# Attention scores written in one burst over four PSUM banks, the upper and lower halves of pairs formed from SBUF, and a new order of a step's work on TensorE and ScalarE

## The chip, the cores and the metric

The kernel runs on one core of a Trainium2 chip. The metric is the device time of one execution in microseconds (us); less is better. The engines are called as the profile calls them: PE (TensorE; PEld is its weight load), DVE (VectorE), ACT (ScalarE), POOL (GpSimd) and SP (the engine that only issues DMAs here).

## What is computed

Three stages, all in fp32:

```
scores = scale * q @ k^T                     # 4 batches x 8 heads, 576 x 576, head size 64
kth    = 32nd largest score of each row      # scores below it are masked out
attn   = softmax(masked scores);  a = attn @ v
x      = a as (2304 tokens, 512)
y      = relu(x @ w_in)**2 @ w_out           # 512 -> 2048 -> 512
out    = y + gate * (relu(y_e @ w1[e]) @ w2[e])   # for tokens with y @ w_skip > 0,
                                             # e = expert (of 8) with the largest logit y @ w_gate
```

## The kernel before

**Tiling.** The attention is 72 steps. A step takes 128 query rows against all 576 keys, for two heads at once (`n` = 0, 1 in the code): 64 steps of kind "pair" and 8 of kind "mixed", which gather the last 64 rows of each head. Eight steps make a group of 256 tokens, so there are 9 groups. The MLP (x to y) runs on a group in 16 units `u` of 128 hidden columns; each unit is `up(u)` (12 matmuls of 256 columns) and, two units later, `down(u)` (6 matmuls of 512 columns). The high and low part of each operand are separate fp32r tiles, which is why there are three products for one. When all y are there, tokens are routed and the experts run tile by tile; the change does not touch that stage.

**One step on the engines.** PE multiplies q and k (`scores_half`, two halves of 288 key columns for both heads). ACT copies each half, scaled, from PSUM to the tile `s_sb` (a ring of 4). DVE finds the 32nd largest value of each row. To halve its work it first forms, from the two halves of a row, the elementwise larger (`upper`) and smaller (`lower`) values, 576 elements each for the two heads (`find_upper`, `find_lower`; one operand is the second half still in PSUM, the other the first half in `s_sb`), and then runs rounds of MAX8 and MATCH_REPLACE8 on them. `mins` and `kth` close a step's search. POOL turns kth into a bias (`set_bounds`), ACT computes from it what lies below (`find_below`), POOL subtracts that (`mask`), ACT exponentiates, DVE inverts the sums (`invert_sums`), POOL multiplies by them (`normalise`), PE transposes the probabilities (`transpose_probs`), ACT copies them back (`copy_transposed`, 1152 columns), PE multiplies by v (`values_product`), and ACT and POOL split the result into x_high and x_low (`copy_values`, `split_x`). For a unit of the MLP, ACT takes relu and g_high, POOL the square and g_low (`square_low`: L644 and L649).

**What sets the order.** No scheduler does: each engine has its own program, written out by hand as a loop over t = 0 to 86, and runs it strictly in that order; semaphores join the engines. In iteration t an engine works on different steps at once. POOL, for instance, does bounds of step t-1, normalise of t-2, split_x of t-3, mask of t-1, then, for t = 1 to 13, its share of splitting the MLP's weights into high and low (`split_out_low` L657, `split_in_low` L664: four pieces at t = 1, three each at t = 2 to 9, one each at t = 10 to 13), then the squares of the two MLP units of t. The MLP runs from t = 10, two units an iteration. In iteration t DVE finishes the search of step t, and forms upper and lower of step t+1 between its third and its fourth round.

PE's iteration before is: first half of the scores of t+1, values of t-3, second half of the scores of t+1, transposes of t-2, both MLP units, and, three times for each group, a share of the routing (`transpose_y`, `route_parts`, `route`). Both halves of the scores use banks 0 and 1 of PSUM in turn, so the second half waits for ACT's copy of the first, and the next step's first half waits until DVE has formed `lower` from the second (the wait on `lower_set`). Transposes use banks 2 to 4, the values part of bank 4, MLP units banks 5 to 7.

## Time and profile before

| | us |
|---|---|
| median of 3 runs | 922.72 |
| lowest and highest of them | 922.64, 923.32 |
| span of the profiled execution | 920.5 |
| of it: attention alone, t = 0 to 9 | about the first 105 |
| of it: attention and MLP together | about 105 to 697 |
| of it: rest of the MLP, routing | about 697 to 790 |
| of it: experts | about 790 to 920 |

A row in order of time gives the start and length in us, the engine, the line, the operation, the tiles it writes and reads with their shapes, and how many equal instructions were merged into it. A row of a group by line gives the count, the busy time, the mean length in ns, then the time for which the engine stood idle before such an instruction and what released it. Matmul lengths overlap, so the distance between starts tells more than their length.

### The profile page before, as it was taken

What the parts mean: (1) busy time and instruction counts of PE and PEld (TensorE: products, weight loads), DVE (VectorE), ACT (ScalarE), POOL (GpSimd) and SP (SyncE); (2) the same over time, 40 slices, a digit from 0 to 9 for tenths busy, and PEclk for the clock granted to TensorE, in tenths of its full rate; (3) what the DMA queues carried; (4) which work ended last, traced back from release to release, by engine and by line L of the source; (5) the groups of instructions that cost most, each with busy time, mean ns of one, the idle gap of its engine ahead of it and who ended that gap; (6) DMA issues with size and microseconds to landing.
All of it is one profiled execution on the core that took longest, in us unless ns stands there. A gap on an engine that the chain in (4) does not pass through costs nothing.

```text
span 920.5 us, 21085 instructions
## 1 busy us (share of the span) xinstructions
PE 885.1 (96%) x6684; PEld 719.2 (78%) x6684; DVE 819.2 (89%) x2584; ACT 658.5 (72%) x1297; POOL 656.6 (71%) x884
## 2 busy tenths in 40 slices
PE   4799899999999999999999999999999999999997
PEld 2677687888888788888788887888878886788886
DVE  6999999999999999999999999999991064888887
ACT  3777787777777778777777777877775322788886
POOL 2999998878887787787888778778787452444432
PEclk7799999999999999999999999999999999999999
DMA  9962533566344658866535455433533675764990
GB/s 332 364 242 95 173 125 124 166 203 193 120 166 142 212 181 280 239 188 229 170 130 169 138 186 171 169 125 125 189 125 114 242 243 208 273 226 154 335 334 23
DMA packets 69750, 175.40 MB, mean 191 GB/s; under 512 B 21298, under 2 KB 26418, under 8 KB 65280
## 3 DMA queue, kind: packets, MB, share of 16 engines
q1 hardware_dynamic: 67568, 168.77, 54.2%
q0 software_dynamic: 1840, 5.06, 1.7%
q8 instruction: 56, 0.92, 0.4%
q14 instruction: 62, 0.51, 0.2%
q10 hardware_dynamic: 224, 0.15, 0.1%
HBM read 154.19 MB, written 21.27 MB: 191 GB/s over the span
## 4 chain that ended last, share of the span: by engine, by line
PE 84%; DVE 11%; POOL 2%; issue 1%; ACT 1%; DMA 0%; DVEq 0%; SPq 0%; POOLq 0%
PE psum L1352 8%; PE psum L1417 7%; PE psum L1418 7%; PE psum L1419 7%; PE psum L1377 7%; PE psum L1434 7%; PE psum L1435 7%; PE psum L1396 7%; PE psum L1436 7%; DVE top L1052 3%; DVE upper L1057 3%; PE psum L1650 2%; PE psum L1619 2%; PE psum L1624 2%; PE psum L1655 2%; PE psum L1658 2%
## 5 line engine op out<-in xcount | busy, mean ns | idle before, releaser
L1052 DVE MAX8 top<-upper 128x8 f32<-128x288 f32 x576 | 238.8, 446 | 0.0
L629 POOL TENSOR_TENSOR s_sb<-s_sb,below 128x576 f32<-128x576 f32 x144 | 203.3, 1434 | 1.5 <-ACT below L801 1.5
L1057 DVE MATCH_REPLACE8 upper<-top,upper 128x288 f32<-128x288 f32 x432 | 187.6, 441 | 0.0
L1417 PE MATMUL psum<-x_high,w_in_high 128*128 128x256 f32 x576 | 168.3, 292 | 1.6 <-POOL x_low L635 1.1
L1418 PE MATMUL psum<-x_low,w_in_high 128*128 128x256 f32 x576 | 161.8, 281 | 0.0
L1419 PE MATMUL psum<-x_high,w_in_low 128*128 128x256 f32 x576 | 161.2, 280 | 0.0
L792 ACT ACTIVATE s_sb<-psum 128x576 f32<-128x576 f32 x144 | 93.8, 651 | 93.7 <-PE psum L1352 84.2
L644 POOL TENSOR_TENSOR square<-relu 128x256 f32<-128x256 f32 x144 | 89.7, 623 | 81.7 <-ACT relu L834 80.9
L649 POOL TENSOR_TENSOR g_low<-square,g_high 128x256 fp32r<-128x256 f32 x144 | 108.4, 753 | 30.3 <-POOL square L644 23.2
L1352 PE MATMUL psum<-k_sb,q_sb 64*128 64x288 f32 x512 | 100.1, 469 | 21.7 <-DVE lower L1043 19.1
L801 ACT ACTIVATE below<-s_sb,steep_kth 128x576 f32<-128x576 f32 x144 | 110.8, 770 | 9.2 <-POOL neg_max L617 8.4
L1067 DVE MAX8 top<-lower 128x8 f32<-128x288 f32 x288 | 115.3, 441 | 0.0
L1434 PE MATMUL psum<-w_ring,g_high 128*128 128x512 f32 x288 | 114.5, 398 | 0.0
L1435 PE MATMUL psum<-w_ring,g_high 128*128 128x512 f32 x288 | 113.5, 394 | 0.0
L1436 PE MATMUL psum<-w_ring,g_low 128*128 128x512 f32 x288 | 113.2, 393 | 0.0
L1417 PEld LDWEIGHTS psum<-x_high,w_in_high 128*128 128x128 f32 x576 | 108.5, 188 | 6.0 <-POOL x_low L635 1.3
L1418 PEld LDWEIGHTS psum<-x_low,w_in_high 128*128 128x128 f32 x576 | 108.7, 189 | 3.2
L809 ACT ACTIVATE s_sb<-s_sb,neg_max 128x576 f32<-128x576 f32 x144 | 110.9, 770 | 0.0
L834 ACT ACTIVATE relu<-psum 128x256 f32<-128x256 f32 x144 | 55.5, 385 | 76.1 <-PE psum L1419 75.0
L1419 PEld LDWEIGHTS psum<-x_high,w_in_low 128*128 128x128 f32 x576 | 108.6, 189 | 0.0
L623 POOL TENSOR_SCALAR s_sb<-s_sb,sums 128x576 f32<-128x576 f32 x144 | 106.3, 749 | 0.0
L1377 PEld LDWEIGHTS psum<-ident,s_sb 128*128 128x128 f32 x576 | 62.1, 142 | 34.0 <-issue 30.2
(213 smaller groups left out, 1848.0 us busy)
## 6 DMA issues: line engine op xcount, KB each, us to landing
w_ring<-w_split SPq DMA_DIRECT2D x144, 512.0 KB, 4.5
weights<-w SPq DMA_DIRECT2D x32, 1024.0 KB, 7.1
v_sb<-v_main SPq DMA_DIRECT2D x48, 256.0 KB, 2.5
w_split<-w_ring SPq DMA_DIRECT2D x16, 512.0 KB, 4.3
k_sb<-kT SPq DMA_DIRECT2D x32, 144.0 KB, 4.5
k_sb<-kT SPq DMA_DIRECT2D x32, 128.0 KB, 4.3
weights<-w_out SPq DMA_DIRECT2D x1, 4096.0 KB, 13.5
weights<-w_in SPq DMA_DIRECT2D x1, 4096.0 KB, 21.1
```

Source lines behind the costliest of these rows:

```text
L629: nc.gpsimd.tensor_tensor(s_sb[:, s % SBUFS, n, 0:S], s_sb[:, s % SBUFS, n, 0:S], below[:, n, :], ALU.subtract).then_inc(masked, 1)
L1052: v.max(top[:, s % 2, n, 8 * r:8 * r + 8], upper[:, s % 2, n, :]).then_inc(upper_step, 1)
L1057: v.match_replace(upper[:, s % 2, n, :], top[:, s % 2, n, 8 * r:8 * r + 8], upper[:, s % 2, n, :], LOWEST).then_inc(upper_step, 1)
L1067: v.max(top[:, s % 2, n, at:at + 8], lower[:, s % 2, n, :]).then_inc(lower_step, 1)
L1352: last = t_.matmul(banks[:, n, :], q_sb[own, a % RING_A, r * P:(r + 1) * P], k_sb[own, a % RING_A, cols], start=True, stop=True)
L1377: t_.transpose(psum[:, 2 + n, k * P:(k + 1) * P], tiles[:, at:at + P], ident[:, :])
L1417: t_.matmul(dst, wh, x_high[:, j % 2, k, :], start=k == 0, stop=False)
L1418: t_.matmul(dst, wh, x_low[:, j % 2, k, :], start=False, stop=False)
L1419: last = t_.matmul(dst, wl, x_high[:, j % 2, k, :], start=False, stop=k == KC - 1)
L1434: t_.matmul(psum[:, 6 + c, :], gh, wh, start=f == 0, stop=False)
L1435: t_.matmul(psum[:, 6 + c, :], gh, wl, start=False, stop=False)
L1436: last = t_.matmul(psum[:, 6 + c, :], gl, wh, start=False, stop=f == FT - 1)
```

## The change

The scores of a step are now written in one burst, half 0 to banks 0 and 1, half 1 to banks 2 and 3, with one semaphore count for the step. ACT copies them in one instruction of 1152 columns (only step 0 is copied by halves). `find_upper` and `find_lower` take both operands from `s_sb` and are plain tensor_tensor max and min. PE no longer waits for `lower_set`; in turn the transposes, which use banks 2 and 3 too, wait until ACT has copied the scores of the step three further on (`scores_copied`), and the burst waits for the copy of the previous transposes. PE's iteration is now: scores of t+1, first MLP unit, routing share, transposes of t-2, second MLP unit, values of t-2. ACT's order follows. The first `up` of a group waits for its last x_low only at its last slice of k. The routing's tiles move from banks 2 and 3 to 0 and 1.

```diff
-        def score_banks(s, half):
-            at = 2 if s == 0 and half == 1 else 0
-            return psum[:, at:at + 2, 0:HALF]
+        def score_banks(half):
+            return psum[:, 2 * half:2 * half + 2, 0:HALF]
...
+            def copy_scores(s):
+                act.wait_ge(scores_done, s + 2)
                 if s >= SBUFS:
                     act.wait_ge(transposed, s - SBUFS + 1)
+                nc.scalar.activation(s_sb[:, s % SBUFS, :, :].rearrange("p n (h c) -> p n h c", h=2),
+                                     psum[:, 0:4, 0:HALF].rearrange("p (h n) c -> p n h c", h=2), ACT.Copy,
+                                     scale=SCALE).then_inc(scores_copied, 1)
...
-                if t + 1 < NS:
-                    copy_scores(t + 1, 0)
+                if 0 <= t - 3 < NS:
+                    copy_values(t - 3)
                 if 0 <= t - 1 < NS:
                     find_below(t - 1, 0)
-                if 0 <= t - 3 < NS:
-                    copy_values(t - 3)
+                    find_below(t - 1, 1)
                 if t + 1 < NS:
-                    copy_scores(t + 1, 1)
...
+                    copy_scores(t + 1)
...
-                v.scalar_tensor_tensor(out=upper[:, s % 2, :, :], in0=score_banks(s, 1), scalar=SCALE,
-                                       in1=s_sb[:, s % SBUFS, :, 0:HALF], op0=ALU.mult, op1=ALU.max).then_inc(upper_set, 1)
+                v.tensor_tensor(upper[:, s % 2, :, :], s_sb[:, s % SBUFS, :, HALF:S], s_sb[:, s % SBUFS, :, 0:HALF], ALU.max
+                                ).then_inc(upper_set, 1)
...
-                v.scalar_tensor_tensor(out=lower[:, s % 2, :, :], in0=score_banks(s, 1), scalar=SCALE,
-                                       in1=s_sb[:, s % SBUFS, :, 0:HALF], op0=ALU.mult, op1=ALU.min).then_inc(lower_set, 1)
+                v.tensor_tensor(lower[:, s % 2, :, :], s_sb[:, s % SBUFS, :, HALF:S], s_sb[:, s % SBUFS, :, 0:HALF], ALU.min
+                                ).then_inc(lower_set, 1)
...
             def transpose_probs(s):
+                pe.wait_ge(scores_copied, min(s + 3, NS - 1) + 2)
                 wait(pe, transposed_copied, s)
+                wait(pe, values_copied, s)
...
+                whole = KC - 1 if ORDER[j] else KC - 2
                 if f == 0:
-                    pe.wait_ge(x_low_done, PER_GROUP * (j + 1))
+                    pe.wait_ge(x_low_done, PER_GROUP * (j + 1) - (2 if ORDER[j] else 1))
...
                 for k in range(KC):
+                    if f == 0 and k == whole:
+                        pe.wait_ge(x_low_done, PER_GROUP * (j + 1))
```

The change's instructions on PE, for a step in which the MLP runs, in the order of its program. Before, L1352 is a score matmul, L1396 the values, L1377 and L1380 the transposes, L1417 the first matmul of an MLP unit, L1434 the first of its second half:

```order
L1352 MATMUL psum<-k_sb,q_sb 128x288 [waits lower_set,scores_copied,kq_loaded0]
L1352 MATMUL psum<-k_sb,q_sb 128x288
L1396 MATMUL psum<-pT_sb,v_sb 64x128 [waits v_loaded2,values_copied,transposed_copied]
L1396 MATMUL psum<-pT_sb,v_sb 64x128 x7
L1396 MATMUL psum<-pT_sb,v_last 64x128 x2
L1352 MATMUL psum<-k_sb,q_sb 128x288 [waits scores_copied]
L1352 MATMUL psum<-k_sb,q_sb 128x288
L1377 MATMUL psum<-ident,s_sb 128x128 [waits probs_done,transposed_copied]
```

After (the same operations are L1353, L1412, L1395, L1438 and L1455; the second piece follows the first MLP unit, the third the second one):

```order
L1353 MATMUL psum<-k_sb,q_sb 128x288 [waits transposed_copied,scores_copied,kq_loaded0]
L1353 MATMUL psum<-k_sb,q_sb 128x288 x3
L1438 MATMUL psum<-x_high,w_in_high 128x256 [waits relu_done]
...
L1395 MATMUL psum<-ident,s_sb 128x128 [waits values_copied,probs_done,transposed_copied,scores_copied]
L1395 MATMUL psum<-ident,s_sb 128x128 x3
L1395 MATMUL psum<-ident,s_sb 128x128 [waits probs_done]
...
L1412 MATMUL psum<-pT_sb,v_sb 64x128 [waits v_loaded2,values_copied,transposed_copied]
```

The two bursts of scores have become one, the transposes stand in the middle of the MLP's work, and they carry a new wait, on `scores_copied`.

On DVE the place of `upper` and `lower` in the program is the same, with other operands. Before:

```order
L1036 SCALAR_TENSOR_TENSOR upper<-psum,s_sb 128x576 [waits upper_step,scores_copied]
L1043 SCALAR_TENSOR_TENSOR lower<-psum,s_sb 128x576 [waits lower_step]
L1052 MAX top<-upper 128x8 [waits upper_step] x2
L1095 RECIPROCAL sums<-sums 128x2 [waits exp_done]
L1052 MAX top<-upper 128x8 [waits upper_set,bias_set]
```

After:

```order
L1046 TENSOR_TENSOR upper<-s_sb 128x576 [waits upper_step,scores_copied]
L1053 TENSOR_TENSOR lower<-s_sb 128x576 [waits lower_step]
L1062 MAX top<-upper 128x8 [waits upper_step] x2
L1105 RECIPROCAL sums<-sums 128x2 [waits exp_done]
L1062 MAX top<-upper 128x8 [waits upper_set,bias_set]
```

Nothing moved here; both inputs are now in SBUF.

On ACT a plain iteration after the change reads as follows (L836 and L837 copy the values, L810 finds what lies below kth, L794 copies the scores, L845 is relu, L818 the exponential, L854 g_high, L827 copies the transposes):

```order
L836 ACTIVATE x_now<-psum 128x128 [waits x_low_done,values_done]
L837 ACTIVATE x_high<-psum 128x128
L810 ACTIVATE below<-s_sb,steep_kth 128x576 [waits masked,bias_set]
L810 ACTIVATE below<-s_sb,steep_kth 128x576 [waits masked]
L794 ACTIVATE s_sb<-psum 128x1152 [waits transposed,scores_done]
L845 ACTIVATE relu<-psum 128x256 [waits squared,unit_up]
L818 ACTIVATE s_sb,sums<-s_sb,neg_max 128x576 [waits probs_done,masked]
L854 ACTIVATE g_high<-relu 128x256 [waits g_low_done,unit_down,relu_done]
L827 ACTIVATE pT_sb<-psum 128x1152 [waits values_done,transposed]
L818 ACTIVATE s_sb,sums<-s_sb,neg_max 128x576 [waits probs_done,masked]
```

Before, the iteration began with the first half of the scores, and the copy of the transposes stood ahead of the first relu:

```order
L792 ACTIVATE s_sb<-psum 128x2x288 [waits transposed,scores_done]
L801 ACTIVATE below<-s_sb,steep_kth 128x576 [waits masked,bias_set]
L825 ACTIVATE x_now<-psum 128x128 [waits x_low_done,values_done]
...
L792 ACTIVATE s_sb<-psum 128x2x288 [waits transposed,scores_done]
L801 ACTIVATE below<-s_sb,steep_kth 128x576 [waits masked]
L816 ACTIVATE pT_sb<-psum 128x1152 [waits values_done,transposed]
L834 ACTIVATE relu<-psum 128x256 [waits squared,unit_up]
```

What moved is that the one copy of the scores now stands behind both `find_below`, so the transposes on PE that wait for it also wait for the kth of that iteration.

## Rows read from the trace of the kernel before

**Rows 1.** Groups by line, 200 to 600: busy us, mean ns; idle before, releaser.

```profile
L649 POOL TENSOR_TENSOR g_low<-square,g_high 128x256 fp32r<-128x256 f32 x83 | 61.1, 737 | 21.7 <-POOL square L644 18.5
...
L644 POOL TENSOR_TENSOR square<-relu 128x256 f32<-128x256 f32 x83 | 51.3, 618 | 39.7 <-ACT relu L834 39.7
...
L816 ACT ACTIVATE pT_sb<-psum 128x1152 f32<-128x1152 f32 x42 | 47.4, 1128 | 0.0
...
L1036 DVE SCALAR_TENSOR_TENSOR upper<-psum,s_sb 128x576 f32<-128x576 f32 x42 | 31.4, 749 | 0.0
...
L1095 DVE RECIPROCAL sums<-sums 128x2 f32<-128x2 f32 x42 | 6.8, 162 | 8.0 <-ACT s_sb L809 8.0
```

**Rows 2.** Stretch 200:300: length, then PE, PEld, DVE, ACT, POOL, clock, DMA.

```profile
200.00:300.00 100.00, 100.00 (x789) 81.91 (x787) 98.62 (x347) 76.41 (x164) 80.37 (x114) 1.00 0.50 163
```

**Rows 3.** In order of time, one step with an MLP: start, length (us), instruction.

```profile
407.12 0.17 DVE L1090 TENSOR_REDUCE kth<-mins 128x2 f32<-128x34 f32 x1
...
411.13 2.83 POOL L629 TENSOR_TENSOR s_sb<-s_sb,below 128x576 f32<-128x576 f32 x2
...
413.50 0.75 DVE L1036 SCALAR_TENSOR_TENSOR upper<-psum,s_sb 128x576 f32<-128x576 f32 x1
...
416.57 0.17 DVE L1090 TENSOR_REDUCE kth<-mins 128x2 f32<-128x34 f32 x1
```

**Rows 4.** In order of time, DVE, a step before the MLP starts.

```profile
65.95 0.16 DVE L1090 TENSOR_REDUCE kth<-mins 128x2 f32<-128x34 f32 x1
...
72.33 0.73 DVE L1036 SCALAR_TENSOR_TENSOR upper<-psum,s_sb 128x576 f32<-128x576 f32 x1
72.99 0.73 DVE L1043 SCALAR_TENSOR_TENSOR lower<-psum,s_sb 128x576 f32<-128x576 f32 x1
...
74.81 0.17 DVE L1083 TENSOR_TENSOR mins<-top 128x34 f32<-128x34 f32 x1
...
75.27 0.16 DVE L1090 TENSOR_REDUCE kth<-mins 128x2 f32<-128x34 f32 x1
```

**Rows 5.** In order of time, POOL, the same step.

```profile
66.20 0.19 POOL L615 TENSOR_SCALAR steep_kth<-kth 128x2 f32<-128x2 f32 x1 [0.65 <-DVE kth L1090]
...
68.37 2.80 POOL L629 TENSOR_TENSOR s_sb<-s_sb,below 128x576 f32<-128x576 f32 x2
71.12 3.75 POOL L664 TENSOR_TENSOR w_in_low<-weights,w_in_high 128x512 fp32r<-128x512 f32 x3
```

**Rows 6.** In order of time, DVE and POOL, second step.

```profile
23.23 4.96 POOL L657 TENSOR_TENSOR w_ring<-weights,w_ring 128x512 fp32r<-128x512 f32 x4
...
27.21 1.03 DVE L1083 TENSOR_TENSOR mins<-top 128x34 f32<-128x34 f32 x1
...
28.54 0.16 DVE L1090 TENSOR_REDUCE kth<-mins 128x2 f32<-128x34 f32 x1
```

**Rows 7.** In order of time, DVE and POOL, routing after the attention.

```profile
750.50 2.29 DVE L1206 TENSOR_TENSOR place_hit<-s_sb,row_iota 128x2048 f16<-128x2048 f32 x1
...
751.81 1.45 POOL L644 TENSOR_TENSOR square<-relu 128x256 f32<-128x256 f32 x1 [1.39 <-ACT relu L834]
...
752.82 0.47 DVE L1207 CAST ahead_values<-s_sb 128x16 f16<-128x16 f32 x1
```

**Rows 8.** By form, 800 to 920: subtraction with both operands in SBUF.

```profile
L1283 DVE TENSOR_TENSOR w_low<-weights,w_high 128x1024 fp32r<-128x1024 f32 x39 | 47.1, 1246 | 2.3 <-ACT w_high L982 2.3
```

**Rows 9.** In order of time, PE, the step at 407.

```profile
410.06 0.76 PE L1352 MATMUL psum<-k_sb,q_sb 64*128 64x288 f32 x4
410.75 1.09 PE L1377 MATMUL psum<-ident,s_sb 128*128 128x128 f32 x8
```

**Rows 10.** In order of time, PE, start of the kernel.

```profile
4.38 2.01 PE L1352 MATMUL psum<-k_sb,q_sb 64*128 64x288 f32 x8 [0.30 <-DMA k_sb<-kT]
...
10.19 1.33 PE L1352 MATMUL psum<-k_sb,q_sb 64*128 64x288 f32 x4 [0.74 <-ACT s_sb L792]
```

More of the change, by code:

```diff
@@ L508, in _ @@
                     if FREED[a - RING_A] == t:
-                        sp.wait_ge(scores_done, 2 * t + 2)
+                        sp.wait_ge(scores_done, t + 2)
                         load_kq(a)
@@ L937, in _ @@
                     square_high(u)
+                if 0 <= t - 2 < NS:
+                    copy_transposed(t - 2)
                 if 0 <= t - 1 < NS:
                     exponentiate(t - 1, 1)
+                for j in range(GROUPS - 1):
+                    if ENDS[j] == t:
+                        copy_yT(j)
+                    if ENDS[j] + 1 == t:
+                        copy_parts(j)
+                    if ENDS[j] + 2 == t:
+                        copy_logits(j)
                 for u in slots[1:2]:
@@ L943, in _ @@
                 for j in range(GROUPS):
[L944 to L949 removed]
+                    if ENDS[j] - 1 == t:
+                        copy_rows(j)
+                if t == ENDS[GROUPS - 1]:
+                    copy_yT(GROUPS - 1)
                 if t == ENDS[GROUPS - 2] + 3:
@@ L1338, in scores_half @@
                 kind, _, _, _, r, a = STEPS[s]
-                if half == 0:
-                    for x in range(a, a + (1 if kind == "pair" else 2)):
-                        pe.wait_ge(kq_loaded[x % RING_A], KQ_COUNT[x])
-                if s > 0:
-                    pe.wait_ge(scores_copied, 2 * s + half)
-                if half == 0:
-                    wait(pe, lower_set, s)
-                banks = score_banks(s, half)
                 cols = slice(half * HALF, (half + 1) * HALF)
@@ L1351, in scores_half @@
                         own = slice(n * HD, (n + 1) * HD)
-                        last = t_.matmul(banks[:, n, :], q_sb[own, a % RING_A, r * P:(r + 1) * P],
+                        last = t_.matmul(psum[:, 2 * half + n, 0:HALF], q_sb[own, a % RING_A, r * P:(r + 1) * P],
                                          k_sb[own, a % RING_A, cols], start=True, stop=True)
@@ L1448, in transpose_y @@
                     for k in range(KC):
-                        last = t_.transpose(psum[:, 2 + c, k * P:(k + 1) * P], rows[:, j % 2, c, k * P:(k + 1) * P], ident[:, :])
+                        last = t_.transpose(psum[:, bank + c, k * P:(k + 1) * P], rows[:, j % 2, c, k * P:(k + 1) * P], ident[:, :])
                     if j == GROUPS - 1 and c == 0:
@@ L1513, in _, with routing_share @@
             keep_clock(5)
-            scores_half(0, 0)
-            scores_half(0, 1)
+            def routing_share(t):
+                for j in range(GROUPS - 1):
+                    if ENDS[j] == t:
+                        transpose_y(j)
+                    if ENDS[j] + 1 == t:
+                        route_parts(j)
+                    if ENDS[j] + 2 == t:
+                        route(j)
+            scores(0)
             for t in range(TIMES):
@@ L1518, in _ @@
                 if t + 1 < NS:
-                    scores_half(t + 1, 0)
-                if 0 <= t - 3 < NS:
-                    values_product(t - 3)
-                if t + 1 < NS:
-                    scores_half(t + 1, 1)
-                if 0 <= t - 2 < NS:
-                    transpose_probs(t - 2)
+                    scores(t + 1)
                 if 2 <= t < FIRST:
                     keep_clock(20)
+                if not slots and 0 <= t - 2 < NS:
+                    transpose_probs(t - 2)
                 for u in slots:
@@ L1536, in _ @@
                         last.then_inc(ahead_transposed, 1)
+                    if u % 2 == 0:
+                        routing_share(t)
+                        if 0 <= t - 2 < NS:
+                            transpose_probs(t - 2)
+                if 0 <= t - 2 < NS:
+                    values_product(t - 2)
                 if t == ENDS[GROUPS - 1]:
@@ L1542, in _ @@
                     up_ahead(0, [0])
-                for j in range(GROUPS):
-                    if ENDS[j] == t:
-                        transpose_y(j)
-                    if ENDS[j] + 1 == t and j < GROUPS - 1:
-                        route_parts(j)
-                    if ENDS[j] + 2 == t and j < GROUPS - 1:
-                        route(j)
+                    transpose_y(GROUPS - 1)
                 if t == ENDS[GROUPS - 1] + 1:
```

81 lines of the change are left out of this document (41 added, 40 removed).

## The prediction

> **What bounds the kernel now.** I read first the stretches, then the groups by line, then one step in order of time. Between 200 and 600 us, where attention and MLP run together, three engines are close to full: PE 100 us of 100, DVE 98.6, POOL 80.4 [rows 2]. The count of `upper` gives the pace: 42 in 400 us, 9.52 us a step on average, plain steps and those with a routing share together [rows 1]. A plain step is 9.45 us, from 407.12 to 416.57 [rows 3]. DVE stands still for only 8.0 us of the 400, before the inversion of the sums [rows 1], 0.19 us a step. So DVE needs 9.52 - 0.19 = 9.33 us for its own work. The first ten steps, without MLP, confirm it: there kth follows kth after 75.27 - 65.95 = 9.32 us [rows 4] with no idle time on DVE. So DVE bounds the first 105 us, PE bounds the next 590 by a hair, and whatever lengthens DVE's step by more than 0.19 us becomes the bound everywhere. After 697 us PE's MLP and then the experts bound; the change leaves these stages alone, and I cost them at nothing.
>
> **The scores on PE.** A half of the scores takes from 410.06 to 410.75, 0.69 us, before the next operation may start [rows 9], two halves 1.38. A burst in one piece stands in the trace once, in step 0 at the lower clock: 2.01 us for eight against 1.33 for four [rows 10], which take 0.76 at the full one [rows 9]. The second four added 0.68 there, and at twice the clock I take 0.34. So the burst costs 0.69 + 0.34 = 1.03, a saving of 0.35 us a step; the ends are 0 (no saving) and 0.45 (the second half costs a third of the first). PE's own work falls from 9.52 to 9.17 on average. Against that stands one new stall. The first `up` of a group needs x_low of step t-3, which POOL now makes in the same iteration, behind bounds and normalise, about 2.3 us after kth. PE reaches that `up` about when kth ends, and its first three quarters last about 1.1 us, so it waits some 1.3 us once in 8 steps, 0.16 a step. PE: 9.33, as much as DVE.
>
> **Upper and lower on DVE.** Their length hardly changes. An operation with both operands in SBUF takes 0.17 us for 34 elements (`mins`, rows 4) and 2.29 for 2048 [rows 7]; on the line between them 1024 elements take 1.21 (measured: 1.246 on average, some of it waiting [rows 8]) and 576 take 0.74, against 0.749 before [rows 1]. The Trainium skill, page "VectorE: DVE Perf Modes", section on the TRN2 errata, gives 120 cycles ahead of the elements for a PSUM source and 58 for SBUF; by that each would be 0.06 us shorter, an estimate of 0.13 a step and 8 us in all if nothing but DVE counted. The row disagrees and decides.
>
> **What DVE and POOL do to each other.** In this trace a DVE operation with two SBUF inputs and a POOL operation do not run together. `mins` of the second step starts at 27.21, while POOL's four splits last from 23.23 to 28.19 [rows 6]; it takes 1.03 us instead of 0.17, and ends about when POOL's fourth ends. That step's kth starts 0.86 us late. It holds the other way too: POOL's square, 618 ns otherwise [rows 1], starts at 751.81 under a `place_hit` that ends at 752.79 and takes 1.45 [rows 7]; and the DVE operation behind, at 752.82, takes 0.47 for 16 elements, while that square runs. So the port changes hands between two DVE operations when POOL has waited. The lost time is the overlap less about 0.13 us. `upper` with one operand in PSUM pays nothing: at 413.50 it runs under `mask` (411.13 to 413.96) for 0.46 us and takes 0.75 as ever [rows 3]. The change gives it a second SBUF operand.
>
> The Trainium skill says the same in "SBUF — State Buffer", section "Who interferes with whom": a DVE instruction with two SBUF inputs contends with a GpSimd one that reads SBUF, and whichever starts first holds the port for its whole length. By this rule the trace agrees.
>
> **Steps without MLP (t = 1 to 9).** Times from the end of kth (66.11): POOL starts at +0.09, ends `mask` at +5.06, and then runs three splits 1.25 apart, to +8.76 [rows 5]; `upper` asks at +6.22, `lower` at +6.88, `mins` at +8.70 [rows 4]. The first split ends at +6.28, which costs `upper` nothing. The second asked at +6.26, after `upper`, and gets the port when `upper` lets it go, at +6.84; it ends at about +8.09, so `lower`, asked at +6.88, loses 8.09 - 6.88 - 0.13 = 1.08. `mins` then asks at +9.78, and the third split is over by then but for its tail. A step costs 9.32 + 1.08. Bounds: without any change of hands POOL still has to fit in 8.67 us of its own and 2 x 0.62 of DVE's, about 10.0, that is +0.67 less what slack absorbs, say +0.3; if the second split came just before `upper` (0.04 us apart), two splits are lost, +2.2. I take 1.08, the one that the order of requests gives: 8 steps of three splits 8.6 us, t = 1 with four another 1. At t = 10 to 13 one split and two MLP units: POOL's 5.0 + 1.3 + 2.7 and DVE's 1.2 give 10.2 against 9.4, 4 x 0.8 = 3. Sum 13 (4 to 22).
>
> **Steps with MLP (58 further ones).** DVE is the later engine, so the rest falls in place behind kth. POOL: `mask` ends at +5.09. ACT: both `find_below` end at +1.9, the scores' copy (1152 columns as pT's, 1128 ns, rows 1) at +3.0, relu at +3.3, the exponential waits for `mask` and ends at +4.5, g_high at +4.9. POOL squares from +5.05 to +5.66 and makes g_low from +5.74 to +6.47 (618 and 737 ns, rows 1). `upper` asks at +6.22 and loses 6.47 - 6.22 - 0.13 = 0.12. PE's transposes start at +3.0 behind the copy and end at +4.2; ACT copies them until +6.0, exponentiates until +6.8, and gives the second relu at +7.05. POOL asks for its square at +7.13, `lower` at +7.0: `lower` is first and loses nothing; the square waits until +7.6, g_low follows until +9.04, `mins` asks at +8.82 and loses 0.09. The step is 9.33 + 0.21 = 9.54. A routing share, three in eight steps, puts up to 1.0 us more on ACT between exponential and second relu, which moves the last g_low under `mins` and past the next kth; I add 0.08 on average. 9.62 against 9.52: 58 x 0.10 = 6 us.
>
> **Sum.** 922.7 + 13 + 6 = 941.7. The profiled execution has a span of 920.5, 2.2 under the median; what lies around the span is unchanged, so the sum goes on the median. Forecast 941 us, own range 928 to 953.
>
> **Rivals.** *Faster.* The requests fall into POOL's gaps (between +6.47 and +7.13 there is one of 0.66 us), or the port is held through both operations, so that what remains is PE's saving: a step then takes the larger of DVE's 9.33 and PE's 9.17 to 9.33. 62 x 0.17 = 10 us less, plus at most 4 early: 913 to 917. For it: the gap exists and ACT's order could place it well. Against it: PE's and ACT's work now hangs on kth through the scores' copy, so POOL's chain keeps its place, and the early steps have no gap at all. *Much slower.* In the MLP steps `lower` comes behind the second unit's square instead of ahead of it. They are 0.13 us apart, and the waits of `upper` push `lower` that way. Then each step loses 0.48 more: 58 x 0.48 = 28, so 969; half of the steps, 955. It decides where `lower` asks later than POOL's second square. The x_low stall and the routing shares, which make PE late, push the square the other way, but under `mins`. *No slowing at all by the port*, because these operations' forms differ from the ones seen: rows 6 and 7 show three forms and both directions, so I hold this for unlikely; it is the faster case. *The change doesn't do what it says* (DVE no longer holding PE): it can't move the steady state, since PE's wait for `lower` is already zero there.
>
> **How the numbers follow.** Forecast 0.52; much slower (953 and above) 0.20; faster 0.22; gains and port losses cancelling 0.06, split over the middle. A measurement of this kernel can tell about 0.2% (1.8 us) from no change. Faster 0.24, same 0.04, slower 0.72. The range goes from 915 to 965: it cuts the lower half of the faster case and the end of the much slower one.
>
> **What will show it.** Right: `upper`, `lower` and `mins` well above 0.75, 0.75 and 0.17 us on average, `lower` near 1.8 in the steps before 100 us; kth to kth about 10.4 us there and 9.6 later; POOL's operations of a step longer by 0.1 to 0.6; PE with idle time ahead of the transposes, released by ACT's copy of the scores; eight score matmuls in about 1.03. Wrong: upper and lower at 0.75 throughout, and a pace of 9.33. It would be wrong in size if the steps with the MLP lock in another order of square and `lower`, or if PE, late by its stall, sets the pace instead of DVE.

## The result, and the profile of the changed kernel

| us | before | changed |
|---|---|---|
| median (lowest, highest), 4 runs each | 923.02 (922.64, 923.47) | 933.89 (933.32, 934.18) |
| span of the profiled execution | 920.5 | 931.5 |
| start of kth, step 0 | 18.35 | 18.11 |
| start of kth, step 9 | 103.25 | 109.94 |
| start of kth, step 13 | 140.56 | 151.07 |
| start of kth, step 71 (the last) | 694.97 | 709.40 |

The changed kernel is slower: ratio 1.0117, 95% interval 1.0103 to 1.0131. The forecast was 941 with a range of 915 to 965.

The starts of kth split the 11.0 us between the two spans. Steps 1 to 9 cost 6.9 more, steps 10 to 13 cost 3.8 more, the 58 steps from 14 to 71 cost 3.9 more (9.626 against 9.559 us a step), the start is 0.2 shorter, and what follows the last kth is 3.4 shorter (222.1 against 225.5).

**The bound has moved to DVE.** First a stretch. The columns are the stretch and its length, the busy time of PE, PEld, DVE, ACT and POOL with their instructions, the granted clock of PE, the share of DMA and GB/s:

```profile
200.00:300.00 100.00, 98.99 (x785) 82.01 (x784) 100.00 (x344) 75.33 (x152) 81.83 (x115) 1.00 0.51 168
```

In [rows 2] PE was the engine without a gap and DVE had 98.6 of 100. Now DVE has no gap, here and in the three stretches up to 600 us, and PE has one of a per cent. The chain that ended last (the work followed back from the last instruction, as shares of the span), in the page of the kernel before and then of the changed one, says the same with other means:

```profile
PE 84%; DVE 11%; POOL 2%; issue 1%; ACT 1%; DMA 0%; DVEq 0%; SPq 0%; POOLq 0%
```

```profile
DVE 66%; PE 27%; issue 5%; DVEq 0%; ACT 0%; DMA 0%; POOL 0%; SPq 0%
```

**Which operations grew.** The groups by line from 200 to 600 us, to be laid beside [rows 1]; the last two numbers ahead of the second bar are busy us and mean ns, behind it stands idle time and its releaser:

```profile
L650 POOL TENSOR_TENSOR g_low<-square,g_high 128x256 fp32r<-128x256 f32 x82 | 62.5, 762 | 6.4
...
L645 POOL TENSOR_TENSOR square<-relu 128x256 f32<-128x256 f32 x82 | 57.8, 705 | 52.1 <-ACT relu L845 52.1
...
L1046 DVE TENSOR_TENSOR upper<-s_sb 128x576 f32<-128x576 f32 x41 | 37.3, 909 | 0.0
...
L1053 DVE TENSOR_TENSOR lower<-s_sb 128x576 f32<-128x576 f32 x41 | 33.3, 812 | 0.0
...
L1093 DVE TENSOR_TENSOR mins<-top 128x34 f32<-128x34 f32 x41 | 10.5, 256 | 0.0
```

`upper` went from 749 to 909 ns, its elements being the same, and `lower` has 812. On the other side of the port `square` went from 618 to 705 ns and `g_low` from 737 to 762. All these operations have the same sizes as before, so the excess is waiting that the profile counts as length.

**The early steps alternate.** From step 1 on, kth follows kth after 10.63, 11.15, 9.33, 10.92, 9.33, 10.91, 9.34, 10.89 and 9.33 us. Before, it followed after 10.19 and 9.42 in the first two of these steps, in which `mins` waited for POOL [rows 6], and after 9.32 or 9.33 from the third on [rows 4]. Two neighbouring steps of the changed kernel in order of time, DVE and POOL together. First the long one:

```profile
95.45 4.76 POOL L665 TENSOR_TENSOR w_in_low<-weights,w_in_high 128x512 fp32r<-128x512 f32 x3
...
96.10 1.23 DVE L1046 TENSOR_TENSOR upper<-s_sb 128x576 f32<-128x576 f32 x1
97.25 1.82 DVE L1053 TENSOR_TENSOR lower<-s_sb 128x576 f32<-128x576 f32 x1
...
100.61 0.17 DVE L1100 TENSOR_REDUCE kth<-mins 128x2 f32<-128x34 f32 x1
100.87 0.19 POOL L616 TENSOR_SCALAR steep_kth<-kth 128x2 f32<-128x2 f32 x1 [0.67 <-DVE kth L1100]
```

and then the short one:

```profile
105.79 5.00 POOL L665 TENSOR_TENSOR w_in_low<-weights,w_in_high 128x512 fp32r<-128x512 f32 x3
...
106.99 0.75 DVE L1046 TENSOR_TENSOR upper<-s_sb 128x576 f32<-128x576 f32 x1
107.66 0.75 DVE L1053 TENSOR_TENSOR lower<-s_sb 128x576 f32<-128x576 f32 x1
...
109.94 0.17 DVE L1100 TENSOR_REDUCE kth<-mins 128x2 f32<-128x34 f32 x1
```

Inside each merged row of three splits (the splitting of the MLP's weights, L665), the second one is what matters. A view of 97.3 to 98.6 shows the second and third of the long step, the second starting at 96.67; in a view of 108.3 to 109 the second of the short step stands alone:

```profile
96.67 3.53 POOL L665 TENSOR_TENSOR w_in_low<-weights,w_in_high 128x512 fp32r<-128x512 f32 x2
```

```profile
107.01 2.53 POOL L665 TENSOR_TENSOR w_in_low<-weights,w_in_high 128x512 fp32r<-128x512 f32 x1
```

In the long step `upper` asks at 96.10, while the first split runs (95.45 to 96.70), and loses 0.49 us. The second split is let in behind `upper`, and `lower` loses 1.07. In the short step the first split is over when `upper` starts (it ends about 107.06, 0.07 of overlap); `upper` and `lower` both run at 0.75, and it is the second split that waits through both: 2.53 us instead of 1.27. POOL is then late. Its three splits end at 110.79, 0.85 us behind the start of kth, where it otherwise begins its next chain 0.26 us behind kth (100.87 after 100.61). So its chain for the next step starts late, its first split falls under the next `upper`, and the next step is a long one. The control below (e2_after_struct) supports this: in its step 5 DVE waited 1.75 us for ACT, POOL caught up meanwhile, and there two short steps followed each other.

### The profile page after: what moved, and what is told of

The parts are those of the page before. It is cut to its first block, busy times and chain, and to the rows that moved or that the text cites. A ratio compares the mean times of both kernels' runs of the same rounds, so it can differ in the third digit from the quotient of the medians.

```text
span 931.5 us, 21036 instructions
## 1 busy us (share of the span) xinstructions
PE 879.7 (94%) x6684; PEld 726.0 (78%) x6684; DVE 844.6 (91%) x2584; ACT 648.2 (70%) x1226; POOL 681.3 (73%) x884
## 4 chain that ended last, share of the span: by engine, by line
DVE 66%; PE 27%; issue 5%; DVEq 0%; ACT 0%; DMA 0%; POOL 0%; SPq 0%
DVE top L1062 21%; DVE upper L1067 18%; DVE top L1077 9%; DVE upper L1046 6%; DVE lower L1082 6%; DVE lower L1053 3%; PE psum L1679 2%; PE psum L1648 2%; PE psum L1653 2%; PE psum L1684 2%; PE psum L1687 2%; PE psum L1657 2%; PE psum L1438 2%; PE psum L1455 2%; PE psum L1457 2%
## 5 line engine op out<-in xcount | busy, mean ns | idle before, releaser
L1438 PE MATMUL psum<-x_high,w_in_high 128*128 128x256 f32 x576 | 175.2, 304 | 8.3 <-POOL x_low L636 8.3
L645 POOL TENSOR_TENSOR square<-relu 128x256 f32<-128x256 f32 x144 | 102.5, 712 | 92.6 <-ACT relu L845 89.7
L810 ACT ACTIVATE below<-s_sb,steep_kth 128x576 f32<-128x576 f32 x144 | 103.9, 771 | 62.4 <-POOL neg_max L618 60.8
L1438 PEld LDWEIGHTS psum<-x_high,w_in_high 128*128 128x128 f32 x576 | 108.5, 188 | 35.9 <-issue 25.4
L818 ACT ACTIVATE s_sb<-s_sb,neg_max 128x576 f32<-128x576 f32 x144 | 110.9, 770 | 27.8 <-POOL s_sb L630 27.7
L650 POOL TENSOR_TENSOR g_low<-square,g_high 128x256 fp32r<-128x256 f32 x144 | 112.9, 784 | 11.3
L1455 PE MATMUL psum<-w_ring,g_high 128*128 128x512 f32 x288 | 113.8, 395 | 0.0
L827 ACT ACTIVATE pT_sb<-psum 128x1152 f32<-128x1152 f32 x72 | 81.2, 1128 | 29.3 <-PE psum L1396 28.5
L1353 PE MATMUL psum<-k_sb,q_sb 64*128 64x288 f32 x512 | 83.5, 446 | 13.1 <-ACT s_sb L794 11.9
L1412 PE MATMUL psum<-pT_sb,v_sb 128*64 128x128 f32 x1024 | 72.0, 284 | 13.4 <-ACT pT_sb L827 13.4
L1412 PEld LDWEIGHTS psum<-pT_sb,v_sb 128*64 128x64 f32 x1024 | 56.1, 139 | 36.0 <-issue 20.0
```

The source lines that it names most:

```text
L650: nc.gpsimd.tensor_tensor(g_low[:, u % RING_G, :], square[:, :], g_high[:, u % RING_G, :].bitcast(F32), ALU.subtract).then_inc(g_low_done, 1)
L1412: last = t_.matmul(values_psum[hd * HD:(hd + 1) * HD, :], v_part, pT_sb[:, at:at + P], start=k == 0, stop=k == KT - 1)
L1438: t_.matmul(dst, wh, x_high[:, j % 2, k, :], start=k == 0, stop=False)
L1455: t_.matmul(psum[:, 6 + c, :], gh, wh, start=f == 0, stop=False)
```

## The experiments

Each set of runs shared a chip and the runs of the kernel before, whose median was 922.82 us beside the first four and 922.65 beside the last two. "Kernel before" and "changed kernel" below are the two of this document. Where an edit only changes where a wait or an operation stands, its diff is cut to that.

**The operands alone (e1_before_sbuf).** The kernel before with the changed operands of `upper` and `lower`, and nothing else of the change:

```diff
-                v.scalar_tensor_tensor(out=upper[:, s % 2, :, :], in0=score_banks(s, 1), scalar=SCALE,
-                                       in1=s_sb[:, s % SBUFS, :, 0:HALF], op0=ALU.mult, op1=ALU.max).then_inc(upper_set, 1)
+                v.tensor_tensor(upper[:, s % 2, :, :], s_sb[:, s % SBUFS, :, HALF:S], s_sb[:, s % SBUFS, :, 0:HALF], ALU.max
+                                ).then_inc(upper_set, 1)
```

(and `lower` with min in the same way)

> The kernel before, with only upper and lower taken from SBUF (tensor_tensor max and min); order and banks as before. Theory A (two SBUF operands make DVE and POOL exclude each other, and that is the loss): slower than before, first ten steps as in the changed kernel (+7 us by t = 9), some 3 more to t = 13, then 0.1 to 0.3 us a step over 58 steps: 933 to 950 us, point 940; upper about 1.25 and lower 1.8 in every second early step. Theory B (the new order, with PE and ACT hanging on kth, is the loss, and SBUF operands cost nothing): 923 us as before, upper and lower 0.75.

Measured: 935.97 us, ratio 1.0142 (1.0125 to 1.0159). Span 935.1. With this edit alone the kernel loses at least as much as with the whole change: 13.2 us against 10.9, though the two intervals overlap. The alternation is there too, with the same lengths, in two neighbouring steps of this kernel (DVE in order of time):

```profile
97.30 1.24 DVE L1036 TENSOR_TENSOR upper<-s_sb 128x576 f32<-128x576 f32 x1
98.46 1.81 DVE L1043 TENSOR_TENSOR lower<-s_sb 128x576 f32<-128x576 f32 x1
...
108.20 0.74 DVE L1036 TENSOR_TENSOR upper<-s_sb 128x576 f32<-128x576 f32 x1
108.86 0.75 DVE L1043 TENSOR_TENSOR lower<-s_sb 128x576 f32<-128x576 f32 x1
```

So PE's new order and the burst are not what makes the kernel slow. After the last kth (709.00) this kernel takes 226.1 us, as the one before does (225.5); the 3.4 us that the changed kernel wins there don't come from its being bound by DVE, since this kernel is bound by DVE too.

**A control (e2_after_struct), and the one factor reversed (e3_after_psum).** `upper` and `lower` can't simply read PSUM in the changed kernel, since the routing and PE's next work would overwrite it. The control has the changed kernel's burst, order and SBUF operands, but PE's burst waits for `lower` again, the routing's tiles are back in banks 2 and 3 and its share, on PE and on ACT, stands behind the second MLP unit. Of this the diff shows PE's part:

```diff
                 if s > 0:
                     pe.wait_ge(scores_copied, s + 1)
+                    wait(pe, lower_set, s)
+                last = scores_half(s, 0)
+                if s > 0:
                     wait(pe, transposed_copied, s - 3)
...
-                last = scores_half(s, 0)
                 if s == 0:
                     last.then_inc(scores_done, 1)
...
                     if u % 2 == 0:
-                        routing_share(t)
                         if 0 <= t - 2 < NS:
                             transpose_probs(t - 2)
+                routing_share(t)
                 if 0 <= t - 2 < NS:
                     values_product(t - 2)
```

> The changed kernel with PSUM laid out so that half 0 of the scores could stay in banks 0 and 1 until DVE has read it: routing tiles back in banks 2 and 3, the routing share behind the second MLP unit, PE's burst waits for lower again. Operands of upper and lower still from SBUF. It is the control for the next kernel. Theory A and B both: as the changed kernel, 934 us, within 3.

Measured: 933.68, ratio 1.0111 (1.0094 to 1.0128), the same as the changed kernel within 0.3 us. In the two traces the stages differ more than the sum: steps 1 to 9 take 1.9 us longer in the control (one of them with that wait of DVE for ACT), steps 10 to 13 take 1.0 less and the 58 behind them 1.3 less. In sum, what PE was freed from, waiting for `lower`, is worth nothing measurable while DVE sets the pace.

The next kernel differs from the control in `upper` and `lower` only: one of their two operands is the first half of the scores, still in PSUM, and since it isn't scaled yet, the instruction is a scalar_tensor_tensor.

```diff
-                v.tensor_tensor(upper[:, s % 2, :, :], s_sb[:, s % SBUFS, :, HALF:S], s_sb[:, s % SBUFS, :, 0:HALF], ALU.max
-                                ).then_inc(upper_set, 1)
+                v.scalar_tensor_tensor(out=upper[:, s % 2, :, :], in0=score_banks(0), scalar=SCALE,
+                                       in1=s_sb[:, s % SBUFS, :, HALF:S], op0=ALU.mult, op1=ALU.max).then_inc(upper_set, 1)
```

> The same as the control, but upper and lower take half 0 from PSUM and half 1 from SBUF (scalar_tensor_tensor), so one operand in SBUF; all results as in the reference. Theory A: the waits at the port go, kth to kth falls to 9.33 us in every stretch, upper and lower 0.75 us; what is left is PE's saving: 912 to 917 us, faster than before and than the control by some 20. Theory B: no change against the control, 931 to 937 us, although upper and lower have 0.75.

Measured: 915.61, ratio 0.992 (0.9903 to 0.9937). This is 18.1 us less than the control, and it beats both kernels. (As in the first run, `lower` is changed with `upper`, with min.) The groups by line from 200 to 600 us show where they went:

```profile
L645 POOL TENSOR_TENSOR square<-relu 128x256 f32<-128x256 f32 x84 | 51.6, 615 | 63.8 <-ACT relu L845 63.8
...
L1053 DVE SCALAR_TENSOR_TENSOR lower<-psum,s_sb 128x576 f32<-128x576 f32 x42 | 31.4, 747 | 0.0
L1046 DVE SCALAR_TENSOR_TENSOR upper<-psum,s_sb 128x576 f32<-128x576 f32 x42 | 31.3, 746 | 0.0
...
L1093 DVE TENSOR_TENSOR mins<-top 128x34 f32<-128x34 f32 x43 | 13.4, 311 | 0.0
```

`upper`, `lower` and `square` are back at the lengths of [rows 1]. An early step of this kernel, DVE and POOL in order of time:

```profile
100.80 3.76 POOL L665 TENSOR_TENSOR w_in_low<-weights,w_in_high 128x512 fp32r<-128x512 f32 x3
102.00 0.75 DVE L1046 SCALAR_TENSOR_TENSOR upper<-psum,s_sb 128x576 f32<-128x576 f32 x1
102.67 0.75 DVE L1053 SCALAR_TENSOR_TENSOR lower<-psum,s_sb 128x576 f32<-128x576 f32 x1
```

Both run beside POOL's splits, and three splits take 3.76 us, as in [rows 5]. `mins`, the operation that still has two SBUF inputs, is the one that still waits: 311 ns against 0.17 us alone, and against 181 ns on average in the kernel before. The pace was expected at 9.33 us in every stretch, and that came out in part: kth follows kth after 9.34 or 9.35 us in steps 3 to 9, but after 9.77 to 9.81 in steps 10 to 13 and after 9.428 on average behind them. In step 10 it is `mins` under POOL's g_low:

```profile
113.67 0.73 POOL L650 TENSOR_TENSOR g_low<-square,g_high 128x256 fp32r<-128x256 f32 x1
113.83 0.62 DVE L1093 TENSOR_TENSOR mins<-top 128x34 f32<-128x34 f32 x1
```

The new order puts that g_low there; before, `mins` took 0.17 in the same steps. So the order has a price at the port too, whatever `upper` and `lower` read.

A rival would be that the form of the instruction decides (tensor_tensor against scalar_tensor_tensor), and not the place of its operands. No run separates the two, but the kernel before has rows for both in its routing. A scalar_tensor_tensor of 16 elements with both inputs in SBUF, started under a g_low, and one behind it with nothing on POOL:

```profile
753.34 0.76 POOL L649 TENSOR_TENSOR g_low<-square,g_high 128x256 fp32r<-128x256 f32 x1
753.42 0.71 DVE L1209 SCALAR_TENSOR_TENSOR s_sb<-onehot,s_sb 128x16 f32<-128x16 f16 x1
754.43 0.18 DVE L1211 SCALAR_TENSOR_TENSOR s_sb<-s_sb 128x16 f32<-128x16 f32 x1
```

and a tensor_tensor with one operand in PSUM, with a square started beside it, both at their own lengths:

```profile
748.96 0.29 DVE L1199 TENSOR_TENSOR s_sb<-psum,s_sb 128x128 f32<-128x128 f32 x1
748.99 0.61 POOL L644 TENSOR_TENSOR square<-relu 128x256 f32<-128x256 f32 x1 [1.84 <-ACT relu L834]
```

So the form alone is not what makes them wait.

**Where the operands cost (e4_psum_early).** The same kernel with the PSUM operand only for the steps below 15, SBUF operands from there on (`lower` in the same way):

```diff
+                if s < 15:
+                    v.scalar_tensor_tensor(out=upper[:, s % 2, :, :], in0=score_banks(0), scalar=SCALE,
+                                           in1=s_sb[:, s % SBUFS, :, HALF:S], op0=ALU.mult, op1=ALU.max).then_inc(upper_set, 1)
+                else:
+                    v.tensor_tensor(upper[:, s % 2, :, :], s_sb[:, s % SBUFS, :, HALF:S], s_sb[:, s % SBUFS, :, 0:HALF], ALU.max
+                                    ).then_inc(upper_set, 1)
```

> The control with the PSUM operand for steps 0 to 14 only, SBUF operands for the other 57. Theory A: the early term (7 us to t = 9, 4 more to t = 14 by the two traces) goes and the later one stays: 923 us, halfway between the two kernels ahead; upper 0.75 before 150 us, about 0.89 after. Theory B: 934.

Measured: 923.8, ratio 1.001 (1.000 to 1.0019). From the first kth to that of step 13 it takes 123.8 us, the control 133.8; from step 14 on both take 9.60 a step. So of the 18.1 us about half, 9.9 (933.68 - 923.8), lies in the first 14 steps, and the other 8.2 (923.8 - 915.61) behind them. The split is good to some 1.5 us: e3_after_psum runs the same work up to there and took 125.3, with a wait of DVE for ACT of 1.68 us in step 2.

**Who gets the port (e5_max_between).** The changed kernel, with one MAX8 moved between `upper` and `lower`; nothing is added:

```diff
                     find_upper(t + 1)
-                    find_lower(t + 1)
                 upper_max(t, 3, 0)
+                if t + 1 < NS:
+                    find_lower(t + 1)
                 upper_max(t, 3, 1)
```

> The changed kernel, with the first MAX8 of the fourth round put between find_upper and find_lower (nothing added or left out). Theory A (two DVE operations back to back keep the port when the first of them did not have to wait, and a POOL operation that asked meanwhile waits for both; a DVE operation that does not need the port, between them, lets POOL in): the alternation of the steps t = 1 to 9 goes; the second split starts behind upper every time, lower asks about 0.4 us later and loses some 0.7 instead of 1.07 in every step, so kth to kth is near 10.0 throughout, kth of step 9 at about 109. In the MLP steps lower asks some 0.4 us later, behind the second unit's square, and loses 0.1 to 0.4 there, the mechanism of the much slower rival in small: mean length of lower above 0.9, 938 to 950 us in all, point 943. Theory B (chance of a few hundredths of a us decides who gets the port, whatever stands between): the alternation stays, with steps of 9.33 and of over 10.5, and the time stays at 934 +-3.

Measured: 941.19, ratio 1.0195 (1.0178 to 1.0212). The alternation is gone: in steps 3 to 9 kth follows kth after 10.34 to 10.36 us, seven times in a row. One of these steps, DVE in order of time, and below it the second and the third split (views of 109 to 109.9 and of 111 to 112):

```profile
108.80 0.74 DVE L1046 TENSOR_TENSOR upper<-s_sb 128x576 f32<-128x576 f32 x1
109.47 0.45 DVE L1062 MAX8 top<-upper 128x8 f32<-128x288 f32 x1
109.84 1.46 DVE L1053 TENSOR_TENSOR lower<-s_sb 128x576 f32<-128x576 f32 x1
...
112.01 0.47 DVE L1093 TENSOR_TENSOR mins<-top 128x34 f32<-128x34 f32 x1
```

```profile
108.84 1.85 POOL L665 TENSOR_TENSOR w_in_low<-weights,w_in_high 128x512 fp32r<-128x512 f32 x1
```

```profile
110.65 1.79 POOL L665 TENSOR_TENSOR w_in_low<-weights,w_in_high 128x512 fp32r<-128x512 f32 x1
```

`upper` starts unhindered, 0.04 us ahead of the second split, as in the short step of the changed kernel. There the split waited through `upper` and `lower`; here it gets in when `upper` is done (1.85 us, 0.6 of it waiting), and `lower` loses 0.71. So theory B has fallen, and theory A's account of who gets the port holds in these steps. It does not hold in all. In step 12 of the changed kernel `upper` starts free, POOL asks 0.07 us later, and yet it gets in between the two:

```profile
137.48 0.73 DVE L1046 TENSOR_TENSOR upper<-s_sb 128x576 f32<-128x576 f32 x1
137.55 1.14 POOL L645 TENSOR_TENSOR square<-relu 128x256 f32<-128x256 f32 x1
138.15 1.16 DVE L1053 TENSOR_TENSOR lower<-s_sb 128x576 f32<-128x576 f32 x1
```

The control has one such step too (`upper` at 119.04). In both it is a square that gets in; the splits and g_low, asking under a free `upper`, waited through both operations every time in the changed kernel, in the control and in e1_before_sbuf.

Theory A's numbers held in part. The step became 10.35 and not 10.0, since the third split, pushed back by `lower`, falls under `mins`, which I had left out: 9.33 + 0.71 + 0.30 = 10.34. The kth of step 9 came at 112.78 and not at 109. In the steps with the MLP the price is 0.13 a step (9.759 against 9.626), in the range expected, but not where I had put it: `lower` averages 0.80 and not above 0.9, and the whole 0.13 stands on `mins`, 384 ns on average against 256. The steps are of two kinds. In about half of them `lower` does come behind the second square and loses 0.12 to 0.13; these take 9.61 to 9.65. In the others `lower` is first, the square waits, and g_low behind it falls under `mins`; nearly all of these take 9.87 and more. One of the second kind, POOL's square at 1.08 instead of 0.61 and `mins` at 0.61:

```profile
386.13 1.08 POOL L645 TENSOR_TENSOR square<-relu 128x256 f32<-128x256 f32 x1 [1.03 <-ACT relu L845]
...
387.45 0.61 DVE L1093 TENSOR_TENSOR mins<-top 128x34 f32<-128x34 f32 x1
```

**The split wait for x_low (e6_psum_whole).** The fastest kernel (one operand in PSUM) with the first `up` of a group waiting for all its x_low at once:

```diff
-                    pe.wait_ge(x_low_done, PER_GROUP * (j + 1) - (2 if ORDER[j] else 1))
+                    pe.wait_ge(x_low_done, PER_GROUP * (j + 1))
...
-                    if f == 0 and k == whole:
-                        pe.wait_ge(x_low_done, PER_GROUP * (j + 1))
```

> The run e3_after_psum (915.6 us, upper and lower with one operand in PSUM, PE and DVE both full) with the one difference that the first up of a group waits for all its x_low before its first matmul, and not only before its last quarter of k. If PE's waits count there as the forecast says (x_low is ready about 2.3 us after kth, PE reaches that up about when kth ends, three quarters of it last 1.1 us), each of the 8 stalls in the loop grows by about 1.1 us, 8 to 9 us in all less what DVE's slack takes up: 919 to 925, point 921. If PE has slack against DVE in that kernel, or x_low is not the wait that ends last, the time stays at 915.6 +-1.5.

Measured: 921.52, ratio to the kernel before 0.9991 (0.9982 to 1.0001), 5.9 us above the kernel without this edit (measured in the other set of runs, whose kernel before was 0.2 us faster), and within the 919 to 925 expected. PE's waits for x_low in that kernel, and then here (us in total, times, longest):

```profile
PE psum L1440 <- POOL x_low L636: 1.4, 2, 1.0
```

```profile
PE psum L1438 <- POOL x_low L636: 10.2, 9, 2.3
```

8.8 us more of waiting cost 5.9 of time, so about a third of it was taken up by PE's slack against DVE. The 1.4 us of the first row is less than forecast: with the wait split, PE hardly waits for x_low in that kernel, where the prediction had 1.3 us in every group. With this wait in one piece the kernel is no faster than the one before: the stall eats what the burst and the order bring, even with `upper` and `lower` off the port.

## Why the prediction was right, step by step

The direction and the mechanism were right. That the number came as near as it did is in part luck: the largest term rests on a timetable whose outcome did not occur, as said below.

**The bound: right.** PE was within a hair of DVE, and any growth of DVE's step above 0.19 us (0.23 by the true average, 9.559 - 9.33) became the time. DVE is full from 200 to 600 us in the changed kernel and heads its chain.

**The mechanism: right, and shown.** `upper` and `lower` with two SBUF operands exclude POOL, those with one in PSUM don't. The operands alone cost 13.2 us on the kernel before (935.97 against 922.82) and 18.1 in the changed structure (933.68 against 915.61). The rival that the port would have no effect has fallen. The "faster" rival, 913 to 917, describes the kernel with one PSUM operand (915.61), and not this one. Even there its terms are not the measured ones: it had 0.17 us a step less over 62 steps, and the trace has 0.13 less over 58 and 3.1 us more in steps 1 to 13.

The Trainium skill's rule ("SBUF — State Buffer", "Who interferes with whom"), by which the operation that starts first holds the port for its whole length, fits the long steps of this trace (`lower` 1.82 us at 97.25). In the short steps the DVE pair held it for two operations (POOL's split 2.53 us at 107.01), longer than the rule says.

**Steps 1 to 9: right in kind, the term too large.** The forecast had 8.6 + 1 = 9.6 us, with `lower` losing 1.08 in every step; measured are 6.9. The step that failed is "the port changes hands between two DVE operations when POOL has waited", taken from [rows 7] as a rule for all cases. The timetable worked out a step in which `upper` starts free and the second split asks 0.04 us behind it, and gave `lower` a loss of 1.08. Such steps exist, they are the short ones, and `lower` loses nothing in them: POOL waits for both operations, and the DVE step is 9.33. The 1.07 stands in the long steps, where `upper` itself had to wait, which the timetable didn't have; the two figures agree because in both one split runs between `upper` and `lower`. The other outcome, the port held through both operations, stood among the rivals as a condition of the faster case. In [rows 7] the second DVE operation starts 0.03 us after the end of the first, while `lower` starts 0.08 before the end of `upper`; whether that is the difference isn't shown. What POOL loses in a short step (1.26 us) comes back as the next step's 10.9, 0.49 for `upper` and 1.07 for `lower`: +1.56 every second step instead of +1.08 in each. Steps 1 and 2 cost 2.2 together, about what was forecast, the first only 0.44, since `mins` no longer waits there; the miss lies in steps 3 to 9, 4.8 us against 7.6.

**Steps 10 to 13: right, with a reservation.** 3 forecast, 3.8 measured, and the excess lengths of `upper`, `lower` and `mins` add up to it. But the same four steps cost 1.9 us more than before in e3_after_psum too, by `mins` alone, so up to half of this would have come without the new operands. In the changed kernel the granted clock of PE was 0.77 from 105 to 110 us and 0.89 to 115, in the control 1.00; steps 10 and 11 took 10.44 and 10.71 us, in the control 9.90 and 10.06. Whether the clock is the reason isn't shown.

**Length of the operations themselves: right.** Unhindered, `upper` with two SBUF operands takes 0.74 to 0.75 us (rows at 106.99 and 107.66), with one in PSUM 0.746 on average. The 0.06 us between the sources, an estimate from the Trainium skill's figures ("VectorE: DVE Perf Modes", the section on the TRN2 errata), doesn't show between the two.

**The steps with the MLP: right in kind, a bit too dear.** 6 us forecast for 58 steps, 3.9 measured. The timetable's `upper`, +0.12, can be read in a step of the changed kernel, DVE and POOL in order of time:

```profile
388.53 0.74 POOL L650 TENSOR_TENSOR g_low<-square,g_high 128x256 fp32r<-128x256 f32 x1
...
388.98 0.89 DVE L1046 TENSOR_TENSOR upper<-s_sb 128x576 f32<-128x576 f32 x1
...
389.80 0.74 DVE L1053 TENSOR_TENSOR lower<-s_sb 128x576 f32<-128x576 f32 x1
```

`g_low` runs under `upper` for 0.29 us, `upper` loses 0.14, and `lower` is free. `mins`, forecast at +0.09, has 0.25 to 0.26 us in most plain steps, against 0.17. A plain step takes 9.55 to 9.57, where 9.54 was worked out. One step of each group takes 10.09 to 10.14: there `upper` waits for a square, g_low gets in behind it, and `lower` takes 1.29. This is the size that the much slower rival had for every step, with another POOL operation. The miss is on the other side of the comparison: I set the average step before at 9.52 from 42 counts in 400 us, and between the kth of steps 13 and 71 it is 9.559. Together with the 9.626 after (9.62 forecast) the difference is 0.067 a step and not 0.10. A count of whole steps in a stretch is too coarse for a difference of 0.1.

**The much slower rival: too dear.** It priced `lower` behind the second square at 0.48 a step. With `lower` asked about 0.4 us later, the cost was 0.13 (9.759 - 9.626). Where `lower` was behind the square, it lost 0.12 to 0.13 and not 0.48, since it asked only when the square was half over (0.35 us behind its start at 179.78); where it was ahead, the waiting fell on the square and then on `mins`.

**The burst on PE: dearer than taken.** In the changed kernel the burst starts at 392.40 and the next matmul follows at 393.57:

```profile
392.40 1.24 PE L1353 MATMUL psum<-k_sb,q_sb 64*128 64x288 f32 x8
393.57 0.39 PE L1438 MATMUL psum<-x_high,w_in_high 128*128 128x256 f32 x1
```

1.17 us against 1.38 before [rows 9]: 0.21 saved, 0.35 forecast, inside the ends of 0 and 0.45. The miss is a misread row. The burst of step 0 at 4.38 [rows 10] was taken as one at the lower clock, but its granted clock was 1.00 and its last two matmuls took 0.41 us, as two do at 410.41. A whole burst at a granted clock of 0.50, the lower of its two levels, is in the changed kernel:

```profile
21.35 2.29 PE L1353 MATMUL psum<-k_sb,q_sb 64*128 64x288 f32 x8 [10.58 <-ACT s_sb L794]
```

The second four add 2.29 - 1.33 = 0.96 there, half of it is 0.48, and 0.69 + 0.48 = 1.17, as measured. It changed nothing here, with DVE as the bound. The two waits that were forecast for PE are there, that of the transposes' weight load for ACT's copy of the scores and that of the first `up` for x_low, in the view of the waits (us in total, times, longest):

```profile
PEld psum L1395 <- ACT s_sb L794: 10.1, 9, 2.7
...
PE psum L1438 <- POOL x_low L636: 8.3, 8, 1.2
```

The wait for x_low is 1.0 us each, where 1.3 was forecast; the one for the copy came only nine times in 72 steps.

**After the attention: not seen.** I costed it at nothing, and it gave back 3.4 us. The two kernels with the old order take 225.5 and 226.1 us behind the last kth, the six with the new one 221.8 to 224.3 (the changed kernel 222.1). The last pT leaves ACT at nearly the same distance from the last kth, 13.2 and 12.2 us. The last x_high, for which the last group's MLP waits, does not. Before, then after (ACT in order of time; the last kth is at 694.97 and 709.40):

```profile
715.22 0.27 ACT L826 ACTIVATE x_high<-psum 128x128 fp32r<-128x128 f32 x1
```

```profile
725.88 0.27 ACT L837 ACTIVATE x_high<-psum 128x128 fp32r<-128x128 f32 x1
```

20.3 us behind it, and 16.5. From this x_high to the end of the span it is 205.3 and 205.6 us, so the whole difference lies ahead of it. In e1_before_sbuf x_high starts 19.9 us behind the last kth, in the other kernels with the new order 16.2 to 17.7. The new order takes the values of a step in the same iteration as its transposes, where the old one took them one iteration later. That it is this and not the shorter burst is only argued: no run separates the two.

**Sum.** 13 + 6 + 0 = 19 forecast against 10.7 + 3.9 - 3.4 - 0.2 = 11.0. Both terms of slowing had the right sign and were 2.3 and 2.1 us too high, and the tail's 3.4 and the start's 0.2 were left out. All four misses point the same way, so they add up to 8 us instead of cancelling. The range, with a width of 50 us, held the result.

## What to carry to other kernels

Where a DVE operation has POOL work beside it, look at its operands and not only at its length: an operand taken from PSUM can be worth more than the PSUM banks that it blocks. Try a change that moves work between engines with its operands kept apart from its order; here burst, order and split wait together gained 7 us (915.6 against 922.8), nearly all of which hangs on the split wait (921.5 without it), and the operands took 18. When two engines exclude each other, their requests are to be put on one time axis for several steps in a row, since the waiting of the one decides where it asks in the next step.

## What the runs showed of the hardware that was not expected

Two DVE operations with two SBUF inputs each, back to back, kept a POOL split or g_low waiting through both when the first had started free (POOL's split at 107.01: 2.53 us instead of 1.27). When the first had itself been waiting for POOL, a POOL operation that asked ahead of the second got in between (`lower` 1.82 us instead of 0.75). Twice a square got in behind a free first operation as well (1.14 us at 137.55 and 1.15 at 119.10 in the control). With one MAX8 between them, 0.37 us from start to start, whose one input is in SBUF, the split got in in all of steps 3 to 9 (1.85 us). What in the arbitration makes the difference between these cases is open. The steps alternated between the two because each case leads to the other.
